# A two-layer MLP inside a fused kernel: first layer as seven quarter products over blocks of 768 tokens, weights streamed per pair of tiles

## The chip, the core and the metric

One NeuronCore of a Trainium2 chip. The metric is the device time of one execution in microseconds. The kernel before took 460.3 us (median of 3 runs, 460.29 to 460.36).

## What is computed

Three stages in fp32: retention (a decayed linear attention over 768 steps, 16 heads), a layer norm with a two-layer MLP and a residual, and a mixture of four causal attention experts. The change is in the second:

```
def _moe_ref(x, g_ln, w_ch1, w_ch2):          # x [2, 768, 512], w_ch1 [512, 2048], w_ch2 [2048, 512]
    mu = np.mean(x, axis=-1, keepdims=True)
    var = np.mean((x - mu) ** 2, axis=-1, keepdims=True)
    xn = (x - mu) / np.sqrt(var + 1e-06) * g_ln
    ch = np.maximum(xn @ w_ch1, 0.0) @ w_ch2
    return (x + ch).astype(np.float32)
```

The stage before it is `y_t = scale * q_t @ state_t`, with `state_t = gamma * state_(t-1) + k_t v_t`. The stage after it is, for each expert, `softmax(causal(q k^T)) v wo`, weighted by a top-2 gate.

## The kernel before, in words

Every engine runs one hand-written instruction stream, and the streams meet at semaphores only. An engine works its stream strictly in order, so a wait holds up all that stands behind it.

**Precision.** An fp32 product is three passes of the faster fp32r type: each operand is split into a rounded high part (`hi`, by ACT or POOL) and the remainder (`lo`, by DVE or POOL), and hi*hi, hi*lo and lo*hi are accumulated (`PASSES`).

**Retention** (iterations `it` 0 to 7, a pair of heads each, HP = 4). SP loads raw k, q and v of an iteration (`load_heads`, L427), three ahead; POOL scales k and q (L301); PE turns them (L625), forms scores (L635), keys times values (L682) and outputs (L648, L655); ACT copies turned tiles and outputs; DVE masks scores and sums states. In its last iterations the layer norm of the first block of tokens is prepared: `first_sum` (head sums), `first_mean` (L665, fp32 matmul with 1/512), `first_centre`, and the split of the normalized x into `xn_t` hi and lo.

**MLP.** Tokens are worked in NB = 3 blocks i of N = 512 (U = 2 tiles of 128 for each of two batches), hidden units in NF = 16 tiles f of 128. The hidden layer lies transposed: units on partitions, tokens along the bank.
- `hidden(i, f)`, L741: 4 k-tiles x 3 passes, 512 columns, into bank f % 2. ACT writes relu to `h_t` hi (L1044), DVE the remainder (L1337).
- `project(i, f)`, L750: second layer, 4 token tiles x 3 passes, 512 columns, accumulated over all f in banks 2 to 5.
- PE's order is hidden(f), project(f-1), hidden(f+1), project(f). It waits for DVE's remainder (`s_hlo`) before project(f).
- All of w1 and w2 is split once by POOL (L514 to L524) and kept.
- DVE, between the remainders of one block: the 32x32 transposes of the block before back to x (`turn_x2`, L1332), of this block's x into token rows (`turn_rows`, L1324), the variance (`moments`, `inverse`, `refine`), and head sums and centring for the next block (`add_heads` L1307, `centre` L1312). The inverse standard deviation is applied at the end, when DVE adds the accumulated banks to `rows` (L1385).
- The last block's result is turned on PE (`turn_last`, L808), split, and goes into the values (L797) and q/k projections (L826) of the experts, which take their turns in a written order.

## Time and profile before

| | before |
|---|---|
| median of 3 runs | 460.3 us |
| profiled execution | 459.9 us |
| its span, first to last instruction | 458.1 us |
| PE busy | 451.3 us |
| DVE busy | 266.1 us |
| ACT busy | 149.9 us |
| POOL busy | 157.0 us |

The profiled execution is 1.8 us longer than its span. PE is TensorE, DVE VectorE, ACT ScalarE, POOL GpSimd, SP the engine that issues most DMAs. A busy matmul is drawn about 0.17 us longer than the interval to the next one, because matmuls overlap; the interval is what one costs. The page says by engine and line where the time lies; the chain of waits says which work ended last; the timelines give single instructions with their start.

### The profile page before, as it was taken

To read this page: it belongs to the slowest core of one execution; us is meant where nothing else is said; L and a number is where in the kernel's file an instruction comes from. 1 tells how busy PE (TensorE), PEld (TensorE's weight loads), DVE (VectorE), ACT (ScalarE), POOL (GpSimd) and SP (SyncE) were. 2 spreads that over 40 slices of the span, in tenths; PEclk is the share of its full clock that TensorE was granted. 3 is DMA by queue.
4 is the path that set the end of the run, shared out by engine and by line. 5 is a ranking of instruction groups with operands and counts; after the bars stand their busy time and mean duration, and the time that the engine had idled before them with its cause. 6 is when DMAs were issued, how large, how long until landed. Compare 5 with 4: busy or idle time off the path is not lost.

```text
span 458.1 us, 7430 instructions
## 1 busy us (share of the span) xinstructions
PE 451.3 (99%) x2762; PEld 391.6 (85%) x2762; DVE 266.1 (58%) x595; ACT 149.9 (33%) x343; POOL 157.0 (34%) x194
## 2 busy tenths in 40 slices
PE   7999999999999999999999999999999999999997
PEld 6899988888888888888888888888999999999875
DVE  4565941485416388732264786143557888887963
ACT  3344431111112111111131111131436677777753
POOL 3754459999600000000003000000813255666650
PEclk9999999999999999999999999999999999999999
DMA  9987314445000000000033000000152533343214
GB/s 211 250 195 178 120 46 139 137 139 137 23 1 0 1 0 0 0 0 0 0 92 71 0 1 0 0 2 0 24 139 70 134 97 97 90 104 88 85 45 163
DMA packets 65759, 32.99 MB, mean 72 GB/s; under 512 B 47552, under 2 KB 61888, under 8 KB 65728
## 3 DMA queue, kind: packets, MB, share of 16 engines
q1 hardware_dynamic: 63072, 31.97, 27.1%
q10 hardware_dynamic: 2656, 0.60, 0.6%
q8 instruction: 19, 0.31, 0.3%
q14 instruction: 12, 0.10, 0.1%
HBM read 19.98 MB, written 3.15 MB: 50 GB/s over the span
## 4 chain that ended last, share of the span: by engine, by line
PE 91%; POOL 3%; SPq 2%; issue 2%; DMA 1%; DVE 0%; ACT 0%; POOLq 0%
PE ps L741 29%; PE ps L750 29%; PE ps L826 7%; PE ps L845 4%; PE ps L797 4%; PE ps L860 4%; PE ps L879 3%; PE ps L648 2%; PE ps L635 2%; PE ps L903 2%; PE ps L655 2%; PE ps L625 2%; SPq L427 1%; DMA raw_q<-in_q 1%; POOL z_t_lo L603 1%
## 5 line engine op out<-in xcount | busy, mean ns | idle before, releaser
L1337 DVE SCALAR_TENSOR_TENSOR h_t_lo<-ps,h_t_hi 128x512 fp32r<-128x512 f32 x48 | 33.2, 692 | 125.1 <-ACT h_t_hi L1044 125.1
L1044 ACT ACTIVATE h_t_hi<-ps 128x512 fp32r<-128x512 f32 x48 | 28.7, 598 | 215.8 <-PE ps L741 215.8
L741 PE MATMUL ps<-xn_t_lo,w_hi 128*128 128x512 f32 x192 | 74.8, 390 | 0.0
L741 PE MATMUL ps<-xn_t_hi,w_hi 128*128 128x512 f32 x192 | 74.8, 390 | 0.0
L741 PE MATMUL ps<-xn_t_hi,w_lo 128*128 128x512 f32 x192 | 74.7, 389 | 0.0
L750 PE MATMUL ps<-w_hi,h_t_lo 128*128 128x512 f32 x192 | 74.7, 389 | 0.0
L750 PE MATMUL ps<-w_hi,h_t_hi 128*128 128x512 f32 x192 | 74.7, 389 | 0.0
L750 PE MATMUL ps<-w_lo,h_t_hi 128*128 128x512 f32 x192 | 74.7, 389 | 0.0
L588 POOL TENSOR_SCALAR a<-a,inv_den,weight 128x768 f32<-128x768 f32 (+5 forms) x48 | 34.1, 721 | 51.5 <-DVE inv_den L1506 25.6
L741 PEld LDWEIGHTS ps<-xn_t_lo,w_hi 128*128 128x128 f32 x192 | 36.0, 188 | 7.9 <-DVE xn_t_lo L1297 0.5
L750 PEld LDWEIGHTS ps<-w_hi,h_t_lo 128*128 128x128 f32 x192 | 36.1, 188 | 7.5
L741 PEld LDWEIGHTS ps<-xn_t_hi,w_lo 128*128 128x128 f32 x192 | 36.0, 188 | 7.5
L741 PEld LDWEIGHTS ps<-xn_t_hi,w_hi 128*128 128x128 f32 x192 | 36.1, 188 | 7.4
L750 PEld LDWEIGHTS ps<-w_lo,h_t_hi 128*128 128x128 f32 x192 | 36.1, 188 | 7.4
L750 PEld LDWEIGHTS ps<-w_hi,h_t_hi 128*128 128x128 f32 x192 | 36.0, 188 | 7.4
L553 POOL TENSOR_SCALAR w_vg_hi<-raw_vg 128x1040 fp32r<-128x1040 f32 x1 | 1.1, 1063 | 119.4 <-DMA raw_wo<-in_moe_wo 119.4
L1099 ACT ACTIVATE a<-a,neg_max 128x768 f32<-128x768 f32 (+5 forms) x48 | 32.2, 674 | 16.5 <-DVE neg_max L1487 16.5
L1324 DVE STREAM_TRANSPOSE rows<-x 32x512 f32<-32x512 f32 x48 | 33.7, 702 | 1.4
L1487 DVE CUSTOM_DVE_ANT_0 a<-ps,masked 128x768 f32<-128x768 f32 (+5 forms) x48 | 27.8, 618 | 0.0
L561 POOL TENSOR_SCALAR raw_qk<-raw_qk 128x256 f32<-128x256 f32 x2 | 0.8, 407 | 76.7 <-PE ps L750 76.7
L860 PE MATMUL ps<-ident,a 128*128 128x128 f32 x168 | 23.6, 276 | 0.8 <-POOL a L588 0.8
L1495 DVE TENSOR_TENSOR a_low_lo<-ps,a_low_hi 128x512 fp32r<-128x512 f32 (+2 forms) x40 | 20.7, 551 | 4.7 <-ACT a_low_hi L1110 4.1
(149 smaller groups left out, 881.6 us busy)
## 6 DMA issues: line engine op xcount, KB each, us to landing
raw_w<-in_moe_w_ch SPq DMA_DIRECT2D x32, 256.0 KB, 2.9
k_twice_hi<-pj_hi SPq DMA_DIRECT2D x32, 96.0 KB, 2.2
k_twice_lo<-pj_lo SPq DMA_DIRECT2D x32, 96.0 KB, 2.2
out_y<-out_sb SPq DMA_DIRECT2D x12, 256.0 KB, 2.0
raw_k<-in_k SPq DMA_DIRECT2D x7, 384.0 KB, 5.0
raw_q<-in_q SPq DMA_DIRECT2D x7, 384.0 KB, 5.6
raw_v<-in_v SPq DMA_DIRECT2D x7, 384.0 KB, 3.5
q_both<-pj_hi SPq DMA_DIRECT2D x16, 96.0 KB, 2.1
```

The lines of the kernel that those rows point to most:

```text
L588: pool.tensor_scalar(a[:, g % AB, c0:c1], a[:, g % AB, c0:c1], inv_den[:, sum_slots(g)][:, w:w + 1], weight[:, u, e:e + 1], ALU.mult, ALU. ...
L741: mm = pe.matmul(ps[:, f % 2, :], w1[a_][:, f, kk, :], xn_t[b_][:, kk, :], start=(kk == 0 and p_ == 0), stop=(kk == KT - 1 and p_ == 2))
L750: mm = pe.matmul(ps[:, 2 + tau, :], h_t[a_][:, f % 2, tau * P:(tau + 1) * P], w2[b_][:, f, :], start=(f == 0 and p_ == 0), stop=(f == NF - ...
L797: mm = pe.matmul(v_bank(t), x2[a_][:, b, kk, c * P:(c + 1) * P], w_vg[b_][:, kk, :], start=(kk == 0 and p_ == 0), stop=(kk == KT - 1 and p ...
L826: mm = pe.matmul(pj_bank(n), w_qk[a_][e][:, kk, :], x2[b_][:, b, kk, half_cols(n)], start=(kk == 0 and p_ == 0), stop=(kk == KT - 1 and p_ ...
L860: mm = pe.transpose(flat(4, 6, s0 + P)[:, s0:s0 + P], a[:, g % AB, s0:s0 + P], ident[:, :])
L1044: act.activation(h_t["hi"][:, f % 2, :], ps[:, f % 2, :], ACT.Relu).then_inc(s_hhi, 1)
L1099: act.activation(a[:, g % AB, c0:c1], a[:, g % AB, c0:c1], ACT.Exp, bias=neg_max[:, 2 * (g % AB) + w:2 * (g % AB) + w + 1], scale=-1.0, ac ...
L1324: dve.transpose(rows[quad(a_), :, :, :, quad(d_)].rearrange("p b k u d -> p (b k) u d"), x[quad(d_), :, U * n:U * n + U, quad(a_)]).then_i ...
L1337: dve.scalar_tensor_tensor(h_t["lo"][:, f % 2, :], ps[:, f % 2, :], 0.0, f32(h_t["hi"][:, f % 2, :]), ALU.max, ALU.subtract).then_inc(s_hl ...
L1487: dve.tensor_tensor_reduce(a[:, g % AB, c0:c1], sc_bank(g, c1)[:, c0:c1], masked[:, NC - 1 - i:NC, :].rearrange("p c t -> p (c t)"), -1.0, ...
L1495: dve.tensor_tensor(a_t("lo", part), at_source(g, part), f32(a_t("hi", part)), ALU.subtract).then_inc(s_atlo, 1)
```

## The change

**Blocks.** Two blocks of 768 tokens (U = 3, a batch's half is W = 384 tokens) in place of three of 512. Hidden tiles are taken in pairs f and f + 8, so there are GROUPS = 16 groups m, eight for each block. x is transposed, centred and quartered (`B11` to `B22`: half of the features by one batch), and w1 of a pair too (`A11` to `A22`: one hidden tile by half of the features).

**First layer.** Group 0 is computed directly in four parts (48 matmuls of 384 columns). Groups 1 to 15 use seven products of quarter blocks, in Winograd's form of Strassen's scheme: S1 to S4 are sums of w1 quarters, T1 to T4 of x quarters. Each product is 2 k-tiles x 3 passes of 384 columns, in banks 0 and 1 in turn. ACT copies the first product to `p1`; DVE makes the sums of products from PSUM and writes the results of parts 22, 21 and 12 back into the bank; then ACT's relu and DVE's remainder follow for each part. The first layer's gain g is now multiplied into the raw weights by ACT (`scale_w1`), not into x.

**Weights.** w1 and w2 of a pair of tiles are loaded for every group, so twice in all, into double buffers. ACT makes high parts of w2 and of three w1 quarters, POOL the four weight sums with their high parts, all seven low parts of w1 and the low parts of w2 (`prepare_w1`, `prepare_w2`). The first two groups' weights are loaded after the heads of retention iteration 5.

**Second layer.** The same 576 matmuls, for six token tiles in banks 2 to 7, in pieces of one or two tiles between the products. The loop over blocks on PE is unrolled.

**DVE's other work** stands in four slots of a group (`beside`): transposes, now of 768 elements (U = 3), token sums, splits and evictions. The x2 splits of the first block come after the last group. `turn_last` turns 384 columns eight times in place of 512 four times, and its units stand before and after values(1) to values(3); the q/k projection of the experts is renamed `project_x2`.

The diff's core (empty lines left out):

```diff
-    U = 2
+    U = 3
...
+    GROUPS = NB * NG
...
+        PRODUCTS = (("A11", "B11"), ("S2", "T2"), ("A12", "B21"), ("S3", "T3"), ("S1", "T1"), ("A22", "T4"), ("S4", "B22"))
+        BANK_ROLE = (A_BANK, B_BANK, A_BANK, B_BANK, A_BANK, B_BANK, A_BANK)
...
+                if it == HP + 1:
+                    load_w(0)
+                    load_w(1)
+            for m in range(2, GROUPS):
+                load_w(m)
...
+            def prepare_w1(m):
+                weight_sum(m, "S1")
+                weight_sum(m, "S2")
+                weight_lo(m, "A11")
+                weight_lo(m, "S2")
+                weight_lo(m, "A12")
+                weight_sum(m, "S3")
+                weight_lo(m, "S3")
+                weight_lo(m, "S1")
+                weight_lo(m, "A22")
+                weight_sum(m, "S4")
+                weight_lo(m, "S4")
+            def prepare_w2(m):
+                for half in range(2):
+                    pool.wait_ge(s_w2hi, 2 * m + half + 1)
+                    pool.tensor_tensor(w2["lo"][:, m % 2, half], raw_w2[:, m % 2, half], f32(w2["hi"][:, m % 2, half]),
+                                       ALU.subtract).then_inc(s_w2, 1)
...
+            for m in range(1, GROUPS):
+                if m + 1 < GROUPS:
+                    prepare_w1(m + 1)
+                prepare_w2(m)
...
+            def product(m, n):
+                a_, b_ = PRODUCTS[n]
+                if n == 0:
+                    pe.wait_ge(s_hlo, part_turn(m - 1, "21") if m > 1 else part_turn(0, "22"))
+                    if m == NG - 2:
+                        pe.wait_ge(s_xc, 2 * KT + KT)
+                elif n == 1:
+                    pe.wait_ge(s_hlo, part_turn(m - 1, "12"))
+                    if m == NG - 2:
+                        pe.wait_ge(s_xc, 2 * KT + 2 * KT)
+                elif n == 2:
+                    pe.wait_ge(s_p1, m)
+                elif n in (3, 5):
...
+                bank = role_bank(m, BANK_ROLE[n])
+                pe.wait_ge(s_w1, w_turn(m, a_))
+                pe.wait_ge(s_xlo, x_turn(m // NG, b_))
+                for kk in range(2):
+                    for p_, (w_, x_) in enumerate(PASSES):
+                        mm = pe.matmul(bank, w_tile(w_, m, a_)[:, kk, :], x_tile(x_, b_)[:, kk, :],
+                                       start=(n in (0, 1, 4, 6) and kk == 0 and p_ == 0), stop=(kk == 1 and p_ == 2),
+                                       skip_group_check=True)
...
+            def project(m, which, tokens):
+                part, b = int(which[0]) - 1, int(which[1]) - 1
+                pe.wait_ge(s_w2, 2 * m + part + 1)
+                pe.wait_ge(s_hlo, part_turn(m, which))
+                for u in tokens:
+                    tau = b * U + u
+                    if m == NG and which in ("11", "22"):
+                        pe.wait_ge(s_x2, tau + 1)
                     for p_, (a_, b_) in enumerate(PASSES):
-                        mm = pe.matmul(ps[:, 2 + tau, :], h_t[a_][:, f % 2, tau * P:(tau + 1) * P], w2[b_][:, f, :],
-                                       start=(f == 0 and p_ == 0), stop=(f == NF - 1 and p_ == 2))
-                    if f == NF - 1:
+                        mm = pe.matmul(acc_bank(tau), h_tile(a_, m, which)[:, u * P:(u + 1) * P], w2[b_][:, m % 2, part, :],
+                                       start=(m % NG == 0 and which in ("11", "22") and p_ == 0),
+                                       stop=(m % NG == NG - 1 and which in ("21", "12") and p_ == 2))
+                    if m % NG == NG - 1 and which in ("21", "12"):
...
+            def next_mean(b):
+                m = NG - 2
+                pe.wait_ge(s_acc, 2 * (HP - 1) + KT - 1)
+                pe.wait_ge(s_hlo, part_turn(m - 1, "21" if b == 0 else "12"))
+                pe.matmul(role_bank(m, A_BANK if b == 0 else B_BANK), f32(mean_of[:, :]), head_half(b), start=True, stop=True,
...
+            def group(m):
...
+                else:
+                    product(m, 0)
+                    project(m - 1, "11", (0, 1))
+                    product(m, 1)
+                    project(m - 1, "11", (2,))
+                    project(m - 1, "21", (0,))
+                    product(m, 2)
+                    project(m - 1, "21", (1, 2))
+                    product(m, 3)
+                    project(m - 1, "22", (0,))
+                    product(m, 4)
+                    project(m - 1, "22", (1, 2))
+                    product(m, 5)
+                    project(m - 1, "12", (0, 1))
+                    product(m, 6)
+                    project(m - 1, "12", (2,))
...
+            for part in FIRST_PARTS:
+                first_hidden(part)
+            for m in range(1, GROUPS):
+                group(m)
+            for which in ("11", "21", "22", "12"):
+                project(GROUPS - 1, which, range(U))
...
+            for m in range(1, GROUPS):
+                first_product(m)
+                if m == NG:
+                    quad_hi(1, "B22")
+                if m + 1 < GROUPS:
+                    scale_w1(m + 1)
+                    weight_hi(m + 1, "A11")
+                    weight_hi(m + 1, "A12")
+                    weight_hi(m + 1, "A22")
+                if m == NG - 1:
+                    quad_hi(1, "B11")
+                hidden_hi(m, "11")
+                if m == NG - 1:
+                    quad_hi(1, "T2")
+                    quad_hi(1, "B21")
+                if m in (NG - 3, GROUPS - 2):
+                    root(m // NG)
+                w2_hi(m, 0)
+                if m == NG - 1:
+                    quad_hi(1, "T3")
+                hidden_hi(m, "22")
+                w2_hi(m, 1)
+                if m == NG - 1:
+                    quad_hi(1, "T1")
...
+            def second_sum(m):
+                dve.wait_ge(s_p1, m)
+                dve.wait_ge(s_h, products_before(m) + 2)
+                dve.tensor_tensor(u2[:, :], role_bank(m, B_BANK), p1[:, :], ALU.add).then_inc(s_u, 1)
+            def third_sum(m):
+                dve.wait_ge(s_h, products_before(m) + 4)
+                dve.tensor_tensor(u3[:, :], role_bank(m, B_BANK), p1[:, :], ALU.add).then_inc(s_u, 1)
+            def fifth_product(m):
+                dve.wait_ge(s_h, products_before(m) + 5)
+                dve.wait_ge(s_u, 3 * (m - 1) + 2)
+                dve.tensor_tensor(u2[:, :], role_bank(m, A_BANK), u2[:, :], ALU.add).then_inc(s_u, 1)
+                dve.tensor_tensor(role_bank(m, A_BANK), role_bank(m, A_BANK), u3[:, :], ALU.add).then_inc(s_c, 1)
+            def fourth_product(m):
+                dve.wait_ge(s_h, products_before(m) + 6)
+                dve.tensor_tensor(role_bank(m, B_BANK), role_bank(m, B_BANK), p1[:, :], ALU.add).then_inc(s_c, 1)
+            def last_product(m):
+                dve.wait_ge(s_h, products_before(m) + 7)
+                dve.wait_ge(s_u, 3 * (m - 1) + 3)
+                dve.tensor_tensor(role_bank(m, A_BANK), role_bank(m, A_BANK), u2[:, :], ALU.add).then_inc(s_c, 1)
...
+            def beside(m, slot):
+                if m in (2, 3):
+                    for q_ in range(8 * (m - 2) + 2 * slot, 8 * (m - 2) + 2 * slot + 2):
+                        turn_rows(0, q_)
+                if m in (4, 13) and slot < 3:
+                    NORMS[m // NG][0](2 * slot)
+                if m in (5, 14) and slot == 0:
+                    NORMS[m // NG][1]()
+                if m in (5, 14) and slot == 3:
+                    NORMS[m // NG][2]()
+                if m == 5 and slot > 0:
+                    add_heads(1, slot)
+                if m == NG - 2:
+                    token_sum(1, T_ORDER[slot])
+                if m == NG - 1:
+                    if slot == 0:
+                        quad_lo(1, "B11")
+                        quad_lo(1, "T2")
+                    if slot == 1:
+                        quad_lo(1, "B21")
+                    if slot == 2:
+                        quad_lo(1, "T3")
+                    if slot == 3:
+                        quad_lo(1, "T1")
+                if m == NG:
+                    if slot == 0:
+                        quad_lo(1, "T4")
+                    if slot == 1:
+                        quad_lo(1, "B22")
+                    if slot > 0:
+                        evict(0, slot - 1)
+                if m in (NG + 1, NG + 2):
+                    first = 8 * (m - NG - 1) + 2 * slot
+                    for q_ in range(first, first + 2):
+                        turn_x2(0, q_)
+                if m in (NG + 3, NG + 4):
+                    first = 8 * (m - NG - 3) + 2 * slot
+                    for q_ in range(first, first + 2):
+                        turn_rows(1, q_)
+            def group(m):
+                second_sum(m)
+                hidden_lo(m, "11")
+                beside(m, 0)
+                third_sum(m)
+                beside(m, 1)
+                fifth_product(m)
+                hidden_lo(m, "22")
+                beside(m, 2)
+                fourth_product(m)
+                hidden_lo(m, "21")
+                beside(m, 3)
+                last_product(m)
+                hidden_lo(m, "12")
+                if m == 5:
+                    for b in range(B):
+                        for kk in range(KT):
+                            centre(1, b, kk)
+                if m == NG:
+                    for tau in range(U, NT):
+                        evict(0, tau)
...
+            def turn_last(n):
+                b, kk = divmod(n, KT)
+                if kk == 0:
+                    pe.wait_ge(s_x2, NT * (NB - 1) + U * (b + 1))
+                if n >= 2:
+                    pe.wait_ge(s_x2lo, KT + n - 1)
+                for u in range(U):
+                    mm = pe.transpose(ps[:, 6 + n % 2, u * P:(u + 1) * P], rows_tile(b * U + u)[:, kk, :], ident[:, :])
```

## Rows read from the trace of the kernel before

**Rows 1.** The page: busy time of each engine, and the granted clock by slice

```profile
PE 451.3 (99%) x2762; PEld 391.6 (85%) x2762; DVE 266.1 (58%) x595; ACT 149.9 (33%) x343; POOL 157.0 (34%) x194
...
PEclk9999999999999999999999999999999999999999
```

**Rows 2.** The chain of waits in order of time: start us, us, what

```profile
59.48 5.62 PE ps L741 x24
65.11 2.72 PE ps L750 x12
67.83 2.72 PE ps L741 x12
...
321.81 1.45 PE ps L797 x12
...
329.35 4.16 PE ps L826 x24
```

**Rows 3.** Timeline of PE around the first token mean (start, us, engine, line)

```profile
57.45 0.70 PE L665 MATMUL ps<-head_sum,mean_of 128*128 128x256 f32 x2
57.98 1.50 PE L655 MATMUL ps<-q_t,state 128*128 128x128 f32 x12
```

**Rows 4.** Timeline where a first-layer piece ends and its result is split

```profile
97.36 0.39 PE L741 MATMUL ps<-xn_t_hi,w_lo 128*128 128x512 f32 x1
...
97.78 0.60 ACT L1044 ACTIVATE h_t_hi<-ps 128x512 fp32r<-128x512 f32 x1 [4.84 <-PE ps L741]
...
98.41 0.69 DVE L1337 SCALAR_TENSOR_TENSOR h_t_lo<-ps,h_t_hi 128x512 fp32r<-128x512 f32 x1 [1.08 <-ACT h_t_hi L1044]
...
99.14 3.65 DVE L1324 STREAM_TRANSPOSE rows<-x 32x512 f32<-32x512 f32 x5
```

**Rows 5.** Groups by form, DVE and ACT: busy us, mean ns | idle before

```profile
L1324 DVE STREAM_TRANSPOSE rows<-x 32x512 f32<-32x512 f32 x48 | 33.7, 702 | 1.4
L1337 DVE SCALAR_TENSOR_TENSOR h_t_lo<-ps,h_t_hi 128x512 fp32r<-128x512 f32 x48 | 33.2, 692 | 125.1 <-ACT h_t_hi L1044 125.1
...
L1476 DVE TENSOR_TENSOR pj_lo<-ps,pj_hi 128x384 fp32r<-128x384 f32 x16 | 8.9, 556 | 11.2 <-ACT pj_hi L1094 10.8
...
L1094 ACT ACTIVATE pj_hi<-ps 128x384 fp32r<-128x384 f32 x16 | 7.8, 487 | 7.5 <-PE ps L826 7.5
```

**Rows 6.** Timelines of DVE and POOL: the same head sum with and without POOL

```profile
110.19 1.57 DVE L1307 TENSOR_TENSOR head_sum<-x 128x512 f32<-128x512 f32 x1
...
197.74 0.66 DVE L1307 TENSOR_TENSOR head_sum<-x 128x512 f32<-128x512 f32 x1
...
109.20 0.63 POOL L522 TENSOR_SCALAR w_hi<-raw_w 128x512 fp32r<-128x512 f32 x1
109.91 1.30 POOL L524 TENSOR_TENSOR w_lo<-raw_w,w_hi 128x512 fp32r<-128x512 f32 x1
111.18 1.06 POOL L514 TENSOR_SCALAR w_hi<-raw_w 128x512 fp32r<-128x512 f32 x1
```

**Rows 7.** Groups by form, POOL

```profile
L524 POOL TENSOR_TENSOR w_lo<-raw_w,w_hi 128x512 fp32r<-128x512 f32 x16 | 20.7, 1292 | 1.3
...
L603 POOL TENSOR_TENSOR z_t_lo<-z_sum,z_t_hi 64x384 fp32r<-64x384 f32 x14 | 14.2, 1018 | 1.2
...
L561 POOL TENSOR_SCALAR raw_qk_more<-raw_qk_more 128x256 f32<-128x256 f32 x2 | 0.8, 409 | 0.0
```

**Rows 8.** Timeline of ACT: four scaled copies of 256 elements

```profile
45.53 1.71 ACT L1004 ACTIVATE xn_t_hi<-centred,g_col 128x256 fp32r<-128x256 f32 x4 [0.24 <-DVE centred L1291]
```

**Rows 9.** Timelines of SP's queue and of POOL in retention

```profile
30.46 0.37 SPq L427 DMA_DIRECT2D raw_v<-in_v  x1
...
43.24 0.83 POOL L301 TENSOR_TENSOR scaled_k<-raw_k,decay_sb 128x384 f32<-128x384 f32 x1 [3.99 <-DMA raw_k<-in_k]
```

**Rows 10.** Stretches: busy time of each engine, clock, DMA share, GB/s

```profile
25.00:30.00 5.00, 4.96 (x80) 4.52 (x78) 2.59 (x5) 1.29 (x4) 3.82 (x5) 1.00 1.06 241
```

**Rows 11.** Timeline of PE where the last x2 tiles are turned

```profile
323.10 1.03 PE L808 MATMUL ps<-ident,rows 128*128 128x128 f32 x8
```

579 lines of the change are left out of this document (321 added, 258 removed).

## Prediction

> **What bounds the kernel now.** First the page: PE is busy 99% of the span, at full granted clock in all forty slices [rows 1]. A share says nothing of who waits for whom, so next the chain of waits. It runs through PE from 59.48 us, where the two MLP layers begin, to 321.81 us, where the values projection follows. In between it is pieces of 12 matmuls in 2.72 us, first layer (L741) and second layer (L750) in turn, end to end [rows 2]. A 512-column matmul thus costs 0.2267 us. There are 1152 of them, 261.1 us, which with two token means fills the 262.3 us of the stage. No other engine costs anything there, and the change must be read as: how much less does PE do, and who can't keep up with a PE that does less.
>
> **PE's work.** The first layer goes from 576 matmuls of 512 columns to 7 products x 6 matmuls x 15 groups + 48 in group 0 = 678 matmuls of 384 columns. The trace has this shape in the later projection: 24 in 4.16 us, so 0.1733 us each [rows 2]. Each of these, too, loads its own weights; the 4.16 us contain that. 678 x 0.1733 = 117.5 us. The second layer stays at 576 x 0.2267 = 130.6 us. Two means as plain fp32 over 384 columns: the 256-column one held PE from 57.45 to 57.98, 0.53 us, so 0.8 us each, 1.6 us [rows 3]. The sum is 249.7 us in place of 262.3: **12.6 us saved**. One group is 42 x 0.1733 + 36 x 0.2267 = 15.44 us; a product is 1.04 us, a token tile of the second layer (three matmuls) 0.68 us.
>
> **What DVE now has in each group.** Before, DVE's part in an f was one subtraction behind ACT's copy, and PE asked for the result only two pieces, 5.4 us, later. The products alternate between two banks only, and a bank is reused once its part has gone through DVE's sum, ACT's relu copy and DVE's subtraction. All these stand in one fixed order on DVE, with other work (beside) in between. Prices: ACT starts 0.20 us after the interval of the last matmul ends (97.36 + 0.227, then 97.78), DVE 0.03 us after ACT's end [rows 4]. A 384-element copy from PSUM takes ACT 0.49 us, a 384-element op of DVE 0.56 us [rows 5]. Count from the end of product 2 (A12 B21) of a group:
> - relu copy and subtraction of part 11: 0.20 + 0.49 + 0.03 + 0.56 = 1.28 us;
> - third_sum 0.56; fifth_product, two sums, 1.12; relu and subtraction of part 22, 0.04 + 0.49 + 0.03 + 0.56 = 1.12;
> - fourth_product 0.56, relu and subtraction of part 21 1.12; last_product 0.56, the same for part 12 1.12.
>
> That is 7.4 us, with some 0.3 us of issue gaps 7.7. Only then may product 1 of the next group overwrite its bank. PE's own way there is 10 tiles and 5 products, 6.8 + 5.2 = 12.0 us. So DVE may have 4.2 us of other work in a group before PE waits; every us above that is on the path.
>
> **Groups with transposes.** turn_rows and turn_x2 now turn 768 elements each, two in each of four slots, in groups 2, 3, 9, 10, 11 and 12. A transpose of 512 takes 0.702 us, and five in a row 3.65, 0.73 each [rows 4, 5]. The 384- and 512-element ops of DVE differ by 0.13 us [rows 5], so 256 elements more are 0.27 us: 1.00 us a transpose. By blocks of 32x32 (24 for 16) it would be 0.73 x 1.5 = 1.09. I take 1.00, since the other ops show a fixed part. Eight are 8.0 us: 7.7 + 8.0 + 0.1 for PE's restart = 15.8 against 12.0, **3.8 us a group, six groups 22.6 us** (20 to 27). The period of such a group would be 19.2 us. DVE is busy 5.6 + 8.0 of it, well under full: what binds is the order, not the load. Before, 80 transposes lay in the gaps of a DVE that PE never waited for.
>
> **Other groups.** Groups 4 and 13 have six bn_stats in three slots, each about 0.7 us as DVE's other 512-element ops [rows 5], 4.1 us before product 0 may start: 0.2 us a group. The change of blocks: in group 5 the inverse (1.2), three add_heads (0.66 x 1.5 = 1.0 each and more [rows 6]) and the refinement (0.8) are 5 us; then eight centrings of 0.56 us stand between part 12 and the products of group 6. next_mean(0) waits for the last head sum some 1.8 us, and product 1 of group 6 starts 2.7 us late in all. Groups 6 to 8 with four token sums, seven splits and six evictions: 2.2 us. Sum 5.3 us (3 to 9).
>
> **Start of the MLP.** Part 11 and 21 of group 0 need only batch 0 and start at 59.3. After 8.3 us of PE, product 0 of group 1 wants the subtraction of part 22, and ahead of it on DVE are the splits of B12 and B22, two subtractions and four token sums, and the split of T2, all of 768 elements, about 1.0 us each (512 in 0.66 [rows 6]). Added up from 60.3, about when the second centrings end (the mean's matmuls start at 57.45 and are 0.3 us longer [rows 3], then four of 0.56), DVE is there at 69.8 where PE could go at 67.6: 2.2 us. But these ops read two SBUF tiles while POOL prepares group 1. With POOL subtracting at 109.91, DVE's head sum of the same shape took 1.57 us, without it 0.66 us [rows 6]. Half of that on four of the seven gives 4 us (2 to 7).
>
> POOL in full: a group costs it eleven 256-element ops of two inputs, four of one, two of 512: 1.29 at 512 and 1.02 at 384 give 0.75 at 256; with 0.41 for the one-input form [rows 7] it is 8.2 + 1.6 + 2.6, with gaps 13.1 of 15.44 us. It begins 2.35 us after product 0, when ACT has scaled the raw weights (four ops in 1.71 us [rows 8]), and delivers the first low half of w2 1.3 us before PE asks. So it hides, with 1.3 us to spare; in the long groups with more.
>
> The Trainium skill, page "SBUF — State Buffer", section "Who interferes with whom", says that a DVE op with two SBUF inputs and a GpSimd op that reads SBUF take turns, the later one waiting for the whole of the other. The trace agrees in 1.57 against 0.66 us. It also says that an op with one SBUF input doesn't contend, so the transposes and PSUM sums keep their prices; by it only the sums and splits can lengthen, by up to 0.75 us each.
>
> **Retention.** 2 MB of weights now go out after the loads of iteration 5, ahead of those of 6 and 7 (k of 6 left right behind 30.46 before). At the 241 GB/s of that time [rows 10] they take 8.5 us. POOL already waited 3.99 us for k of iteration 7, which it got at 43.24, and PE turned it from 49.8 on [rows 9]. Counting 2.0 + 1.2 + 0.8 MB from 31 us, q of 7 lands near 48.8, and its last scaling ends near 51: 1.5 us late (0 to 4). ACT's extra copies there lie in its idle time.
>
> **After the MLP.** 24 turns in place of 16 (1.03 us for 8, pipelined, so 0.9 us more [rows 11]), and the last two now stand directly ahead of the first projection, with copy and subtraction of 0.49 and 0.56 us in the open: 1.4 us. 2.3 us (1 to 3.5). POOL's split of w_vg follows its last w2 but ends some 6 us before PE asks; the x2 splits lie under the last 36 matmuls (8.2 us).
>
> **Sum** against the profiled execution's 459.9 us (span 458.1; 0.4 under the median): 459.9 + 1.5 - 12.6 + 4 + 22.6 + 5.3 + 2.3 = **483.0 us**. All low ends together give 473, all high ends 499.
>
> **Rivals.**
> - *PE stays the bound.* If DVE's chain does not hold PE in the six groups nor at the change of blocks (shorter ops, or overlap that I don't see), 27.9 us go: 455.1 us, faster. For it: DVE would be busy about 13.6 of 15.4 us. Against it: every link is a wait written in the program, and each price is a row. It decides where the work beside the sums is under 4.2 us; it is 8. Chance 0.09.
> - *Half of it.* The chain holds, but by less: between the two times, 0.05, of which 0.01 falls within 0.2% of before.
> - *POOL sets the pace.* If the turns taken at the port add 3 us to POOL's group, it passes its 1.3 us of slack, and PE waits 1.7 us or more in each of the nine short groups, w2's low half being last: 483 + 15 to 20 = 500 us. The page named above is the rule behind it. For: POOL runs at 85% of the group, and its one-input op went from 0.63 to 1.06 us beside a DVE sum [rows 6]. Against: DVE has ops with two SBUF inputs in only a few groups. 0.08.
> - *As forecast*, 0.78.
>
> **Numbers.** The forecast alone spans 473 to 499, and its ends need every term at its end. Range 471 to 498: it leaves out the faster cases and the upper half of POOL's. Within 0.2% of before, about what the measurement can tell from no change: 0.01. Faster 0.09, slower 0.90.
>
> **What would show it.** L741's successor: 384-column matmuls 0.173 us apart, and in all 678. PE idle in the MLP of some 32 us, released by DVE's subtraction of parts 21 and 12; groups 2, 3 and 9 to 12 lasting 19 us, groups 1 and 15 15.5 us; DVE transposes at 1.0 us. POOL busy 12.4 us a group. I am wrong if PE is dense in groups 2 and 3, if the releaser there is POOL or ACT, or if short groups last over 16 us.

## The result, and the profile after

The changed kernel takes 492.5 us (median of 4 runs, 489.1 to 493.6) against 460.3: 1.0685 of the time before, 95% interval 1.0631 to 1.0738. Its profiled execution took 493.0 us, with a span of 491.3; that of before was 459.9, with 458.1. The forecast was 483.0, with a range of 471 to 498. So 33.2 us are to be accounted for, where 23.1 were forecast.

First the page of the kernel after, the same parts as [rows 1]:

```profile
PE 455.9 (93%) x2872; PEld 405.7 (83%) x2872; DVE 321.7 (65%) x669; ACT 219.6 (45%) x519; POOL 293.2 (60%) x391
...
PE   8998988989799798999789788999989999999997
...
PEclk9999998999999898999999999999999999999999
...
L882 PE MATMUL ps<-xq_B_hi,w_hi 128*128 128x384 f32 x90 | 31.7, 352 | 14.0 <-DVE h_t_lo L1577 14.0
...
L1564 DVE STREAM_TRANSPOSE rows<-x 32x768 f32<-32x768 f32 x32 | 31.0, 969 | 0.9
```

PE's share fell from 99 to 93%, its slices show holes over the whole MLP, and the clock line has three 8s where before it had none. They lie at the start of group 1, at the token means of group 5 and in group 7, and the stretches there say what an 8 hides (busy us and count of PE, PEld, DVE, ACT and POOL, then the granted clock, DMA share and GB/s):

```profile
75.70:79.00 3.30, 3.30 (x11) 2.73 (x10) 2.34 (x4) 2.35 (x6) 0.23 (x1) 0.51 0.56 159
164.60:167.50 2.90, 2.88 (x6) 1.98 (x7) 2.19 (x5) 0.49 (x1) 0.00 (x0) 0.50 0.95 314
188.30:191.80 3.50, 3.50 (x11) 3.14 (x10) 0.56 (x1) 1.17 (x3) 3.33 (x6) 0.51 0.73 218
```

Each is about 3 us at the lower level of 1.2 GHz and costs 1.6 us, 4.8 in all. The waits of the same kernel (who waited, for whom, us in total, times, longest) name the engine that holds PE. `L882` is the products of the first layer, `L897` the second layer, `L910` the token means of the next block, `L1577` is `hidden_lo`, DVE's subtraction:

```profile
PEld ps L882 <- DVE h_t_lo L1577: 28.6, 23, 3.8
```

The stages are bounded by the first matmul of the first layer and the first of the values projection. Timeline of PE in the kernel after (start us, us, engine, line):

```profile
62.87 0.42 PE L847 MATMUL ps<-xq_B_hi,w_hi 128*128 128x384 f32 x1
...
351.71 0.28 PE L972 MATMUL ps<-w_vg_hi,x_hi 128*128 128x260 f32 x1
```

So retention ends 3.4 us later than at 59.48 [rows 2], the MLP takes 288.8 us in place of 262.3 (+26.5), and what follows takes 139.6 in place of 136.3 (+3.3).

Inside the MLP I read the start of product 0 of each group off PE's timeline. The periods of groups 1 to 14 are, in us: 17.3, 17.6, 19.1, 17.1, 23.6, 13.9, 20.3, 15.8, 18.1, 19.1, 19.0, 19.1, 17.1, 15.7. Undisturbed is 15.69; by the written order group 5 is 2.1 us longer and group 6 as much shorter, since the token means and some of the second layer stand ahead of product 0 there. A group with transposes delays product 0 and product 1 of the next one. Timelines of PE's weight loads and of DVE at the start of group 4 (the bracket is the idle time just before, and who ended it):

```profile
129.02 0.19 PEld L882 LDWEIGHTS ps<-xq_B_hi,w_hi 128*128 128x128 f32 x1 [2.12 <-DVE h_t_lo L1577]
132.74 0.19 PEld L882 LDWEIGHTS ps<-xq_T_hi,w_hi 128*128 128x128 f32 x1 [1.45 <-DVE h_t_lo L1577]
...
125.28 1.97 DVE L1564 STREAM_TRANSPOSE rows<-x 32x768 f32<-32x768 f32 x2
127.29 0.57 DVE L1601 TENSOR_TENSOR ps<-ps,p 128x384 f32<-128x384 f32 x1
128.41 0.56 DVE L1577 SCALAR_TENSOR_TENSOR h_t_lo<-ps,h_t_hi 128x384 fp32r<-128x384 f32 x1 [0.56 <-ACT h_t_hi L1263]
```

Two transposes (1.97 us) stand ahead of part 21's sum (L1601), and 0.05 us after its subtraction ends PE starts. The two waits, 2.12 and 1.45 us, less 0.04 each of an undisturbed load, are 3.5 us a group.

### The profile page after: what moved, and what is told of

It is laid out like the page before. It is cut to its first block, busy times and chain, and to the rows that moved or that the text cites. A ratio compares the mean times of both kernels' runs of the same rounds, so it can differ in the third digit from the quotient of the medians.

```text
span 491.3 us, 8368 instructions
## 1 busy us (share of the span) xinstructions
PE 455.9 (93%) x2872; PEld 405.7 (83%) x2872; DVE 321.7 (65%) x669; ACT 219.6 (45%) x519; POOL 293.2 (60%) x391
## 4 chain that ended last, share of the span: by engine, by line
PE 56%; DVE 21%; POOL 10%; issue 5%; ACT 4%; DMA 2%; SPq 1%; POOLq 0%; DVEq 0%
PE ps L897 14%; PE ps L882 12%; PE ps L1002 7%; DVE rows L1564 6%; PE ps L1021 4%; PE ps L1036 3%; PE ps L1055 3%; ACT h_t_hi L1263 3%; DVE h_t_lo L1577 3%; DVE x L1572 3%; POOL w_lo L614 3%; PE ps L972 2%; PE ps L746 2%; PE ps L1079 2%; PE ps L736 2%
## 5 line engine op out<-in xcount | busy, mean ns | idle before, releaser
L1263 ACT ACTIVATE h_t_hi<-ps 128x384 fp32r<-128x384 f32 x64 | 31.3, 491 | 164.4 <-DVE ps L1596 67.5
L897 PE MATMUL ps<-w_hi,h_t_hi 128*128 128x512 f32 x192 | 77.0, 401 | 2.4 <-POOL w_lo L635 2.4
L897 PE MATMUL ps<-w_hi,h_t_lo 128*128 128x512 f32 x192 | 77.1, 402 | 0.0
L897 PE MATMUL ps<-w_lo,h_t_hi 128*128 128x512 f32 x192 | 76.8, 400 | 0.0
L1577 DVE SCALAR_TENSOR_TENSOR h_t_lo<-ps,h_t_hi 128x384 fp32r<-128x384 f32 x64 | 35.6, 556 | 60.6 <-ACT h_t_hi L1263 60.6
L635 POOL TENSOR_TENSOR w_lo<-raw_w,w_hi 128x512 fp32r<-128x512 f32 x32 | 41.3, 1310 | 14.5 <-ACT w_hi L1211 14.5
L614 POOL TENSOR_TENSOR w_lo<-w_sum,w_hi 128x256 fp32r<-128x256 f32 x60 | 47.8, 807 | 2.5
L882 PE MATMUL ps<-xq_T_hi,w_hi 128*128 128x384 f32 x120 | 41.3, 344 | 6.0 <-DVE h_t_lo L1577 6.0
L882 PE MATMUL ps<-xq_B_hi,w_hi 128*128 128x384 f32 x90 | 31.7, 352 | 14.0 <-DVE h_t_lo L1577 14.0
L897 PEld LDWEIGHTS ps<-w_hi,h_t_lo 128*128 128x128 f32 x192 | 36.6, 191 | 8.0
L897 PEld LDWEIGHTS ps<-w_hi,h_t_hi 128*128 128x128 f32 x192 | 36.9, 192 | 7.6 <-POOL w_lo L635 3.1
L882 PE MATMUL ps<-xq_T_lo,w_hi 128*128 128x384 f32 x120 | 40.9, 341 | 0.0
L882 PE MATMUL ps<-xq_T_hi,w_lo 128*128 128x384 f32 x120 | 40.7, 339 | 0.0
L897 PEld LDWEIGHTS ps<-w_lo,h_t_hi 128*128 128x128 f32 x192 | 36.7, 191 | 4.5 <-issue 0.3
L1338 ACT ACTIVATE a<-a,neg_max 128x768 f32<-128x768 f32 (+5 forms) x48 | 32.2, 674 | 16.7 <-DVE neg_max L1794 16.7
L614 POOL TENSOR_TENSOR w_lo<-raw_w,w_hi 128x256 fp32r<-128x256 f32 x49 | 38.2, 783 | 0.0
L882 PEld LDWEIGHTS ps<-xq_B_hi,w_hi 128*128 128x128 f32 x90 | 16.9, 188 | 21.0 <-DVE h_t_lo L1577 19.6
L882 PEld LDWEIGHTS ps<-xq_T_hi,w_hi 128*128 128x128 f32 x120 | 22.9, 191 | 11.3 <-DVE h_t_lo L1577 8.9
L1564 DVE STREAM_TRANSPOSE rows<-x 32x768 f32<-32x768 f32 x32 | 31.0, 969 | 0.9
L882 PE MATMUL ps<-xq_B_lo,w_hi 128*128 128x384 f32 x90 | 30.6, 340 | 0.0
```

The source lines that it names most:

```text
L614: pool.tensor_tensor(w_tile("lo", m, name), w_source(m, name), f32(w_tile("hi", m, name)), ALU.subtract).then_inc(s_w1, 1)
L635: pool.tensor_tensor(w2["lo"][:, m % 2, half], raw_w2[:, m % 2, half], f32(w2["hi"][:, m % 2, half]), ALU.subtract).then_inc(s_w2, 1)
L882: mm = pe.matmul(bank, w_tile(w_, m, a_)[:, kk, :], x_tile(x_, b_)[:, kk, :], start=(n in (0, 1, 4, 6) and kk == 0 and p_ == 0), stop=(kk ...
L897: mm = pe.matmul(acc_bank(tau), h_tile(a_, m, which)[:, u * P:(u + 1) * P], w2[b_][:, m % 2, part, :], start=(m % NG == 0 and which in ("1 ...
L1263: act.activation(h_tile("hi", m, part), part_bank(m, part), ACT.Relu).then_inc(s_hhi, 1)
L1338: act.activation(a[:, g % AB, c0:c1], a[:, g % AB, c0:c1], ACT.Exp, bias=neg_max[:, 2 * (g % AB) + w:2 * (g % AB) + w + 1], scale=-1.0, ac ...
```

## The experiments

All but two leave the computation whole. The measured group periods say more than the total where an edit is worth 1 to 4 us: in the seven profiled kernels that load the first weights where the kernel after does, the MLP starts anywhere from 62.9 to 65.6 us, and in those with later loads from 60.2 to 66.8. The quoted expectations name kernels by number: e1 has fewer transposes, e2 slot 0 placed earlier, e3 later loads, e4 ACT's earlier scaling, e5 the order at the start, e6 the work spread, e7 all of it, e8 no seven products, e9 the loads behind all heads.

**Fewer transposes.** In groups 9 to 12 each transpose turns one token tile of three, so that two thirds of block 1's turning is left out.

```diff
-    dve.transpose(rows[..., :, ...], x[..., U * n:U * n + U, ...])
+    dve.transpose(rows[..., 0:u_, ...], x[..., U * n:U * n + u_, ...])   # u_ = U if n == 0 else 1
```

> The changed kernel, but the transposes of block 1's groups (turn_x2 of block 0 and turn_rows of block 1, groups 9 to 12) turn one token tile of three, 256 elements in place of 768; the other tiles of x and rows keep old values, so the output is not the reference's. Groups 2 and 3 stay as they are, as a control. Chain theory (PE waits for DVE's fixed order; a group has 4.2 us for work beside the sums): a small transpose is 0.73 - 0.27 = 0.46 us, eight are 3.7 us, under 4.2, so groups 10 to 12 last 15.5 to 15.7 us in place of 19.1, groups 2 and 3 as before, and four times 3.5 us go: 492.5 to about 478.5. Rival, the port or POOL's pace holds PE: transposes read one tile and don't matter, groups 9 to 12 stay above 17 us, and the time stays over 488.

Measured 478.3 us (1.0428, 1.0374 to 1.0481). Groups 10 to 14 took 15.7 us each, while groups 2 to 4, unchanged, took 17.6, 19.1 and 17.1 as before. One stretch of both kernels (busy us and count of each engine), first with the small transposes, then the kernel after:

```profile
240.00:290.00 50.00, 50.00 (x250) 44.90 (x249) 29.03 (x58) 19.03 (x44) 38.62 (x56) 1.00 0.21 64
```
```profile
240.00:290.00 50.00, 43.63 (x211) 37.29 (x210) 33.77 (x47) 16.50 (x39) 32.35 (x48) 1.00 0.15 45
```

PE is dense as soon as DVE's work beside the sums is short, with GpSimd (POOL) and ACT doing more per us than before. So the transposes in this order are the cause of those groups' length, and the price of two thirds of them is 13.5 us in groups 9 to 13 (92.4 to 79.0 us). The MLP stage is 16.8 us shorter; the other 3.3 lie in groups the edit doesn't touch, above all groups 5 and 7, where this execution had no stretch at the lower clock.

**The same work, one slot placed earlier.** Slot 0's two transposes go between `second_sum` and part 11's subtraction, where DVE is idle for 2.3 us.

```diff
     second_sum(m)
+    if early: beside(m, 0)
     hidden_lo(m, "11")
-    beside(m, 0)
+    if not early: beside(m, 0)
```

> The changed kernel with the same instructions, but in groups 2, 3 and 9 to 12 the two transposes of slot 0 stand between second_sum and the subtraction of part 11, where DVE's trace shows 2.3 us of idle time while PE computes product 2. Chain theory: 2.0 us of the 8.0 leave the chain, each of the six groups takes 19.1 - 2.0 = 17.1 us, 12 us less in all, about 480.5. Rival, DVE's load as such: its busy time is the same, so no change (within 1 us). Rival, the two transposes are counted from product 2's end in any case because the subtraction comes later by as much: no change, and the group stays at 19.1.

Measured 488.3 us (1.0605, 1.0557 to 1.0653): far less than expected. The full groups took 18.45 us in place of 19.1, and of the two waits only the first shrank, 2.12 to 1.67 us. My model had one chain per group with one allowance. In fact `third_sum` (L1589) has to wait for product 3 whatever was done before, so the chain begins again there. DVE in group 3 of this kernel:

```profile
120.96 0.56 DVE L1589 TENSOR_TENSOR u<-ps,p 128x384 f32<-128x384 f32 x1 [1.35 <-PE ps L882]
```

In the kernel after it started without a wait at 120.51, 0.87 us after product 3 had ended. From the end of product 3 the sums, copies and subtractions up to part 12 take 6.4 us and PE's own way 9.6: slots 1 to 3 may hold 3.2 us in all, and the six transposes still there are 5.9, so 2.7 us too much; the groups are 2.8 longer than 15.69.

**The same work, spread.** Every piece of DVE's work is kept. A slot ahead of part 11 takes two transposes, the four others one each, over groups 1 to 3 and 9 to 13, and the `bn_stats`, head sums, refinement and splits are spread in the same way.

```diff
+    spread_steps([(turn_rows, 0, q_) for q_ in range(NQ)],
+                 [(1, 0), (1, 1), (1, 2), (1, 3)] +
+                 [(m_, s_) for m_ in (2, 3) for s_ in (PRE, PRE, 0, 1, 2, 3)])
```

> The changed kernel with all of DVE's work kept but spread: two steps in the idle stretch between second_sum and the subtraction of part 11, one in each slot; transposes in groups 1 to 3 and 9 to 13, variance in 4, 5 and 14, 15, head sums in 4 and 5. Chain theory: every group then has at most 4.0 us on the chain (5.0 in groups 12 and 13), so the six long groups fall from 19.1 to about 15.7 and the head sums no longer hold the mean: 21 + 3 us less, about 468.5. Rival, load: DVE's busy time is unchanged, 492. If port contention counts, 5 to 10 us of the gain stay out, in groups 5 to 8.

Measured 473.8 us (1.0301, 1.0256 to 1.0346), 18.7 less than the kernel after, by order alone. The chain of waits of this kernel in groups 2 and 3 is PE and nothing else:

```profile
95.83 1.06 PE ps L882 x6
96.89 1.39 PE ps L897 x6
```

Groups 2 to 4 and 10 to 12 took 15.7 us. Left were 3.8 us ahead of group 1 and its slow matmuls (17.3), 5.4 in group 5 (of which group 6 gives 1.9 back, and 1.3 is the token means' own work), 4.2 in group 7 and 1.7 in the periods of groups 13 and 14, behind the crowded groups 12 and 13. Those I had counted at less, hence 473.8 and not 468.5.

**Without the seven products.** The first layer direct (8 quarter products) in all groups; blocks of 768 and the streamed, per-pair split weights stay.

```diff
-    def product(m, n): ...          # 42 matmuls a group, sums on ACT and DVE
+    def part_of_group(m, n): ...    # 48 matmuls a group, 12 then 9 of the second layer, in turn
```

> One part undone: blocks of 768 tokens, streamed weights, quarters and DVE's slots as in the changed kernel, but the first layer is computed directly in all groups (four parts of 12 matmuls), with no seven products, no sums of weights, tokens or products. The output is the reference's. PE: 90 matmuls of 384 columns more, 15.6 us. Chain theory: DVE's links between PE and PE are then one copy and one subtraction, with 6 us between a part's end and its bank's next use, so all stalls in groups go (about 27 us), those of the start too (5 us): 492.5 + 15.6 - 32 = about 476, PE dense in all groups, groups of 16.5 us. If blocks of 768 and streaming were at fault, not the products, it would stay above 488. If the products had paid for themselves, it would be slower than the changed kernel.

Measured 474.7 us (1.0315, 1.0287 to 1.0342). Its chain of waits:

```profile
99.89 2.08 PE ps L870 x9
101.97 2.10 PE ps L838 x12
```

From 64.1 to 334.2 us PE is dense but for 0.9 us at the first token mean, with 0.175 us a first-layer matmul and 0.231 a second-layer one. So blocks of 768 and streamed weights account for 14.4 us of the 32.2 by themselves: 7.7 in the MLP stage (270.0 against 262.3), the rest at its two ends. The other 17.8 belong to the seven products as they are ordered, although they save 90 matmuls, 15.7 us of PE's work. The transposes stand here in the same slots as in the kernel after and hold nobody, so it takes them together with the sums of products to hold PE.

**Later loads.** The two first sets of weights go out one head later each, and ACT scales the first of them one step later.

```diff
-    if it == HP + 1:
-        load_w(0)
-        load_w(1)
+    if it >= HP + 2:
+        load_w(it - HP - 2)
```

> The first two sets of streamed MLP weights are loaded one head later (behind the attention's heads 6 and 7), and ScalarE scales the first set one step later. If the streaming's loads cause the late start of the MLP (first product at 62.87 us against the 59.3 of the kernel before, with the sixth head's k issued at 35.62 instead of 30.87), the first product returns to 59.5 to 60.5 and the time falls by 2.5 to 3.5 us, to about 489 to 490. Rival, ScalarE's four extra copies delay it: their count is unchanged, the first product stays at 62 to 64 and the time at 492.5.

Measured 488.8 us (1.0626, 1.0601 to 1.0651), and the MLP started at 60.2. PE's weight loads in the kernel after, where iteration 6 is turned, first; then POOL in this kernel, which has k of 6 at 35.44 (42.47 in the kernel after), and k of 7 at 46.20:

```profile
44.92 0.31 PEld L736 LDWEIGHTS ps<-ident,scaled_q 128*128 128x128 f32 x3 [1.26 <-POOL scaled_q L311]
45.71 0.31 PEld L736 LDWEIGHTS ps<-ident,scaled_k 128*128 128x128 f32 x3 [0.48 <-POOL scaled_k L311]
46.50 0.31 PEld L736 LDWEIGHTS ps<-ident,scaled_q 128*128 128x128 f32 x3 [0.48 <-POOL scaled_q L311]
```
```profile
35.44 0.83 POOL L311 TENSOR_TENSOR scaled_k<-raw_k,decay_sb 128x384 f32<-128x384 f32 x1 [2.56 <-PE ps L792]
...
46.20 0.83 POOL L311 TENSOR_TENSOR scaled_k<-raw_k,decay_sb 128x384 f32<-128x384 f32 x1 [6.73 <-DMA raw_k<-in_k]
```

The loads were the cause. The edit moved ACT's scaling as well, but its copies delayed nothing in the kernel after: ACT had them done by 40.5 us and stood idle until 42.7, while POOL waited 8.9 us for k of 6 to land.

**ACT scales set 7 earlier**, ahead of group 6's products.

```diff
+    if m == NG - 2: scale_w1(m + 1)
     first_product(m)
...
-    scale_w1(m + 1)
+    if m != NG - 2: scale_w1(m + 1)
```

> One step of ScalarE is moved: the scaling of set 7 of the streamed weights stands ahead of the products of group 6's first layer instead of behind them. If ScalarE's order is what made GpSimd start those sums at 173.1 us, the gaps of 2.5 and 0.6 us ahead of the second layer at 187 and 221 us go, with the half-clock matmuls behind the first: minus 3 to 4.5 us, about 488.5. Rival, GpSimd is simply too slow beside VectorE there: the gap stays and the time is 492.

Measured 491.5 us (1.0663, 1.0610 to 1.0715), not told apart from the kernel after by its time, since its profiled execution started the MLP at 65.6. Where POOL begins with set 7, first in the kernel after, then here:

```profile
173.09 0.74 POOL L602 TENSOR_TENSOR w_sum<-raw_w 128x256 f32<-128x256 f32 x1 [9.94 <-ACT raw_w L1196]
...
185.73 2.52 POOL L635 TENSOR_TENSOR w_lo<-raw_w,w_hi 128x512 fp32r<-128x512 f32 x2
```
```profile
169.94 0.73 POOL L602 TENSOR_TENSOR w_sum<-raw_w 128x256 f32<-128x256 f32 x1 [4.09 <-ACT raw_w L1196]
...
205.67 0.19 PEld L897 LDWEIGHTS ps<-w_hi,h_t_hi 128*128 128x128 f32 x1 [1.25 <-POOL w_lo L635]
```

Counted from the start of the MLP, POOL begins 5.8 us sooner. The 2.5 us gap ahead of the second layer in group 7 went, groups 6 and 7 together took 31.1 us in place of 34.2 (half of that is the stretch at the lower clock, which went with it), and a wait of PE for POOL came back as 1.25 us one group later. The MLP stage is 2.5 us shorter. The cause is confirmed, the gain halved by what comes next.

**Order at the start.** In group 1 the splits that product 0 needs go ahead of the sums T3 and T4.

```diff
     hidden_lo(0, "21")
-    token_sum(0, "T3")
-    token_sum(0, "T4")
     quad_lo(0, "T2")
     hidden_lo(0, "22")
-    quad_lo(0, "T3")
     hidden_lo(0, "12")
+    token_sum(0, "T3")
+    token_sum(0, "T4")
+    quad_lo(0, "T3")
```

> In group 1 the split of T1 and of the x block (what product 0 of the group waits for) is placed on VectorE and ScalarE ahead of the later sums T3 and T4. If queueing order is the cause of the 3.8 us gap before group 1, the gap falls under 1 us, the matmuls at the lower clock level behind it go, group 1 takes 15.7 to 16 us instead of 17.34, and the time falls by 4 to 5 us to about 488. Rival, the operations are slowed by GpSimd's at the same time, whatever their order: the gap stays over 2.5 us and the time at 491 to 492.

Measured 489.2 us (1.0669, 1.0618 to 1.0719); its runs spread up to 493.5, which the ratio contains, so its time is not told apart from the kernel after either. The gap shrank from 3.8 to 2.0 us and not to under 1, and group 1 took 15.79 us in place of 17.34. Those 1.6 us are the clock. PE in the kernel after, behind its gap, against the weight load behind the shorter gap here:

```profile
76.38 0.63 PE L897 MATMUL ps<-w_hi,h_t_hi 128*128 128x512 f32 x1
76.80 0.63 PE L897 MATMUL ps<-w_lo,h_t_hi 128*128 128x512 f32 x1
```
```profile
74.70 0.19 PEld L882 LDWEIGHTS ps<-xq_B_hi,w_hi 128*128 128x128 f32 x1 [2.01 <-DVE h_t_lo L1577]
```

After 3.8 us of idleness the 512-column matmuls are 0.43 us apart, the 1.2 GHz level, and later 0.231 again. Behind the 2.0 us gap none is. This order took away about half of the gap; what the other 2.0 us are, order again or operations slowed by GpSimd, it does not show.

**All of it.** The three edits above, the spreading, the values of head 4 ahead of the first two projections in the tail, and two crowded slots relieved (the root's refinement of block 0 moves to group 8, the last transposes to group 14).

> Nothing is taken out of the computation; the order is changed: e3, e4, e5 and e6 together, the values of head 4 ahead of the first two projections in the tail, the root of block 0 and the extra transposes one step away from their crowded slots. From e6's 473.8 us: minus 3 to 4.5 for the MLP's start, 4.5 for group 1's gap and clock, 3.1 for group 7, 1.7 for the tail, 1.8 for the switch group, 1.7 for groups 12 and 13, which gives 456 to 459, against 460 for the kernel before. If the seven-product layer costs TensorE more than its count (the matmuls 0.231 apart in the second layer), or the gaps move elsewhere, it stays at 463 to 468.

Measured 458.8 us (11 runs, 457.9 to 460.5), 0.9970 of the kernel before, 0.9961 to 0.9980. The profiled execution is the slowest of the eleven, 460.5 us. Nothing of the computation is left out. The page and what still waits on PE in its MLP:

```profile
PE 445.8 (97%) x2872; PEld 403.0 (88%) x2872; DVE 321.8 (70%) x669; ACT 219.1 (48%) x519; POOL 294.9 (64%) x391
...
PE   7999998999999999999999999999999999999997
...
PEld ps L881 <- DVE h_t_lo L1578: 2.0, 1, 2.0
PEld ps L896 <- POOL w_lo L634: 1.7, 2, 1.4
```

DVE, ACT and POOL have the same work as in the kernel after; PE waits for it only where shown. Groups 5 and 6 together are still 1.3 us over twice 15.69, which is the two token means' own matmuls, 0.65 us each, and no wait. The MLP takes 256.9 us, 5.5 less than before. It starts 3.2 us later and the rest takes 2.9 us more. The tail edit brought 1.1 us of the 1.7 expected: behind the start of the values it takes 139.2 us in place of the spread kernel's 140.3. That is only 0.4 less than in the kernel after, since both kernels with the work spread lose 0.8 us earlier, at the turns between the first values.

**Loads behind all heads.** On top of the last kernel: both first sets of weights are loaded behind the last head, set 8 is scaled early as well, and part 22 is split ahead of T2 in group 1.

```diff
-    if it >= HP + 2:
-        load_w(it - HP - 2)
-for m in range(2, GROUPS):
+for m in range(GROUPS):
     load_w(m)
...
-    if m == NG - 2:
+    if m in (NG - 2, NG - 1):
         scale_w1(m + 1)
...
-    quad_lo(0, "T2")
     hidden_lo(0, "22")
+    quad_lo(0, "T2")
```

> e7 with three more changes of order: both first sets of MLP weights are loaded behind all of the attention's heads (as the kernel before did), ScalarE scales set 8 ahead of group 7's products as it does set 7, and in group 1 the split of the hidden part 22 stands ahead of that of T2. If these places are what they look like in e7's trace (MLP at 62.7 us with k of head 7 waited for 6.8 us; 1.4 us gap at 186.8; 2.05 us gap ahead of group 1), minus 0.5 to 2, 1.4 and 1.0 us: 455 to 456 against 458.8, so 0.9% faster than the kernel before. Rival: the gaps move to the next wait, and the time stays within 0.5 us of 458.8.

Measured 462.5 us (1.0050, 1.0033 to 1.0066), slower by 3.7. ACT and PE's weight loads of this kernel:

```profile
50.50 1.71 ACT L1193 ACTIVATE raw_w<-raw_w,g_col 128x256 f32<-128x256 f32 x4 [3.90 <-DMA raw_w<-in_moe_w_ch]
52.24 1.34 ACT L1199 ACTIVATE w_hi<-raw_w 128x256 fp32r<-128x256 f32 x4
...
56.80 0.51 ACT L1163 ACTIVATE q_t<-ps 128x384 f32<-128x384 f32 x1
...
56.60 1.69 PEld L743 LDWEIGHTS ps<-q_t,k_t 64*128 64x128 f32 x20 [4.14 <-ACT q_t L1163]
```

k of 7 came 3.5 us sooner, but ACT stood at the scaling of weights not yet landed, and behind it in ACT's order is q of the last head, for which PE waited 4.1 us. The MLP began at 66.8 in place of 62.7. A load moved must be followed by its consumer's place on every queue.

**Weights prepared thin.** From group 3 on, scaling, sums and splits of the weights work on 16 columns, so the products use weights largely left from an earlier group.

```diff
-    pool.tensor_tensor(w_tile("lo", m, name), w_source(m, name), f32(w_tile("hi", m, name)), ALU.subtract)
+    pool.tensor_tensor(w_tile("lo", m, name)[:, :, 0:c_], ..., ALU.subtract)   # c_ = P if m < 3 else 16
```

> e7, but from group 3 on the scaling, sums and splits of the streamed weights on ScalarE and GpSimd work on 16 columns instead of 128 or 512 (the products use weights that are largely left from an earlier group; loads and all matmuls stay). Whether the preparation beside TensorE is what holds the second layer's 512-column matmuls at 0.231 us apart (before: 0.2267) and a plain group at 15.69 us. If it is, the group falls to 15.4 us, 3.5 us in all, besides the 1.4 us gap of group 8: about 454. If the spacing belongs to the mix of 384- and 512-column matmuls, the group stays at 15.69 and only the gap goes: about 457.

Measured 456.7 us (0.9929, 0.9913 to 0.9945). The same stretch, first with thin weights, then the full kernel beside it, as stretches:

```profile
208.00:300.00 92.00, 92.00 (x458) 82.64 (x457) 64.23 (x102) 22.10 (x78) 19.34 (x87) 1.00 0.24 67
```
```profile
208.00:300.00 92.00, 92.00 (x459) 82.68 (x458) 65.26 (x97) 33.21 (x77) 68.74 (x98) 1.00 0.24 67
```

With 19 us of POOL's work in place of 69, PE does the same 458 matmuls in 92 us. The preparation does not slow PE's pace; it costs the gap in group 8 (here 15.69 us, there 17.03), and the start of this execution was 1.7 us earlier.

**The start once more.** The all-in-one kernel with only the last edit's split order.

```diff
-    quad_lo(0, "T2")
     hidden_lo(0, "22")
+    quad_lo(0, "T2")
```

> e7 with the one change of e9 that removed its gap: ahead of group 1 the hidden part 22 is split before T2, on ScalarE and on VectorE. The loads of the weights stay where e7 has them. e9 had no gap ahead of group 1 but lost 4 us where ScalarE stood waiting for the later loads ahead of the last head's q. If that is how e9's loss comes about, this kernel keeps e7's start (MLP at 61 to 63 us), loses the 2.05 us gap ahead of group 1 down to about 1, and takes 457.5 to 458, 0.4 to 0.5% faster than the kernel before. Rival: the new order in group 1 is what cost e9 its time (its group 2 took 16.68 us instead of 15.69), and this one stays at 459 or above.

Measured 458.7 us (0.9967, 0.9955 to 0.9979). The start is at 60.2 here, so the kernel with the loads behind all heads lost its start by where it loads the weights, as its ACT and PE show above, and not by the order of the splits. But the gap of 2.05 us ahead of group 1 only turned into two of 1.05 and 1.02 us in groups 1 and 2, one waiting for ACT's copy of product 0, the other for POOL's low half of w2. The edit gains nothing.

## Why the prediction was right, and where its size was off

The direction and the main cause were as forecast, and 492.5 us lies inside the range (its high ends add up to 498, not 499); the excess over the forecast is 10.1 us of the 33.2. Term by term, in us, forecast and then measured:

- *PE's work*: -12.6, measured -9.2. The stage of 288.8 less what is over the undisturbed periods (37.0) leaves 251.8, and the two token means add 1.3 (0.65 each, forecast 0.8). Counts were right. The price of a matmul was not: pieces of six take 1.39 and 1.05 us in the chain of waits, which is 0.2315 and 0.1745 in place of 0.2267 and 0.1733, so a group is 15.7 and not 15.44.
- *Start of the MLP stage*: 4, measured 5.5: a gap of 3.8, in the middle of the step's 2 to 7, and 1.6 for matmuls at the lower clock level, which no step contained. (The step's own prices, seven operations of 1.0 and three of 0.56 us from 60.3, give 69.0 and not 69.8.)
- *Groups with transposes*: 22.6, measured 20.7 over groups 2 to 4 and 9 to 13 (their periods less 15.69). This step carries the loss, and the small transposes show it. Its chain was right in content and wrong in form: I counted one allowance of 4.2 us from product 2 on, but the chain restarts at product 3 with 3.2 us. For the order as it was, both give nearly the same, 3.8 and 3.5 a group (2.7 from the six transposes behind `third_sum`, 0.8 because slot 0's two make it late). That agreement was luck. For the order that I tried next, the first model was wrong by 8 us.
- *Change of blocks*, groups 5 to 8: 5.3 (3 to 9), measured 9.5 (10.8 less the means' 1.3). This is the term that was mis-sized most. Of the 9.5, 6.3 are waits, near the forecast, but not all of them where I had put them, and 3.2 are the clock, which I had put at nothing. In group 5 the token mean waited for the last head sum, 3.1 us where I had 1.8. One reason is in DVE's timeline of the kernel after, where operations of 6 elements took 0.85 and 1.18 us, and 0.17 once POOL was done. DVE, then POOL, then PE's weight loads:

```profile
161.10 0.85 DVE L1510 TENSOR_TENSOR newton<-rstd 128x6 f32<-128x6 f32 x1
161.99 1.18 DVE L1511 TENSOR_TENSOR newton<-newton,veps 128x6 f32<-128x6 f32 x1
163.21 0.17 DVE L1512 TENSOR_SCALAR newton<-newton 128x6 f32<-128x6 f32 x1
163.41 0.17 DVE L1513 TENSOR_TENSOR rstd<-rstd,newton 128x6 f32<-128x6 f32 x1
...
160.64 2.51 POOL L635 TENSOR_TENSOR w_lo<-raw_w,w_hi 128x512 fp32r<-128x512 f32 x2
...
164.62 0.50 PEld L910 LDWEIGHTS ps<-head_sum,mean_of 128*128 128x128 f32 x2 [3.12 <-DVE head_sum L1559]
```

  In groups 7 and 8, 3.3 us were lost where I had 2.2 for DVE's sums and splits, and 2.9 of them were waits for POOL. A PE held ahead of group 6 holds ACT's copy of product 0, behind which ACT's scaling of set 7 stands; POOL got it 9.9 us after it was free, and then PE waited for POOL (2.5 and 0.6 us). I had said that POOL hides with more room in long groups. It doesn't when its input comes through the engine that was held. Behind the waits of 3.1 and 2.5 us came two of the three stretches at the lower clock, 1.6 us each. The kernel with the later loads has the same gap in group 7 without one, and 8.9 us over four undisturbed groups in place of 10.8.
- *Retention*: 1.5 (0 to 4), measured 3.4 in this execution, and 4.3 to 6.1 in the six other profiled kernels with the same loads, so the range was too low. I let only the last iteration be late. In fact k of iteration 6, issued at 35.6 in place of 30.9, came 7 us later and PE stood 2.5 us at its turning already.
- *After the MLP*: 2.3 (1 to 3.5), measured 3.3. From the last turns to the first projection it took 2.2 us, of which 1.7 is a wait, in place of the 1.4 forecast.

The terms of the MLP make 26.5, and with retention 3.4 and the tail 3.3 the sum is 33.2. Of the 10.1 us by which the forecast fell short, the clock is 4.8, in three places, and the price of a matmul 3.4; retention, the tail and the waits of groups 5 to 8 are 3.9, and the steps that came out lower take 2.0 off.

*What was to show it.* PE waited for DVE's subtractions (28.6 us, 3.8 of them for part 22 at the start), and otherwise 3.1 us for the head sum and 3.1 for POOL: right in the main, with POOL as a releaser in group 7 that was not foreseen. Full transposing groups at 19.1 us, forecast 19.2: right. Transposes 0.97 us: right. Group 15 and the group after the last transposes at 15.7 where 15.5 was said; group 1 at 17.3, wrong, through the clock. POOL as the pace of short groups: the rival fell, since they run at 15.7 with PE dense, and with thin weights at the same. *PE stays the bound* fell as well for this order, but the spread kernel shows that it is a rival that depends on order alone: all the work is there and PE is dense in the same groups.

Where the gain would have gone in any case: with DVE's order mended the seven products save 13.1 us of MLP (256.9 against the 270.0 of the direct form, whose order was not mended and which has 0.9 us of a gap), while blocks of 768 with streamed weights cost 7.7 us there (270.0 against 262.3) and some 6 more at both ends. That is why the best version is only 0.3% faster than the kernel before.

The Trainium skill, page "SBUF — State Buffer", section "Who interferes with whom", which the prediction drew on, has DVE and GpSimd take turns where a DVE operation has two SBUF inputs. The 6-element operations above agree with it: with two SBUF inputs they took 0.85 and 1.18 us, ending at 161.95 and 163.17 where POOL's two subtractions end at 161.93 and 163.15, and 0.17 us (L1513) when POOL was idle. It decides more than the "up to 0.75 us" which I allowed each split: a tiny operation can wait for a whole one of POOL.

## What to carry to other kernels

Where an engine works in one fixed order between two uses of a bank, price the stretch from each point at which the chain restarts, not the group as a whole, and spread the other work so that no stretch exceeds its own allowance: here 18.7 us came back with no work removed. When something is held, follow what stands behind the held instruction on its engine, here ACT's scaling, then POOL, then PE one group later; and move a load only together with the place where its consumer waits. Removing one gap in such a chain often shows the next at half the size, so test the sum of edits and not each edit's share.
